# Trainium2: the head of a mixture-of-experts stage reordered by high and low parts, with unread products on TensorE ahead of it

## The reference, cut to what matters

```python
logits = x @ w_gate                                   # 512 -> 8
local_gate = sigmoid(x @ w_local)
for each sequence b, each row s:
    fresh = argmax(logits[b, s])
    e = fresh if s == 0 or local_gate[b, s] < 0.5 else prev_e
    p = softmax(logits[b, s])
    h = maximum(x[b, s] @ w1[e], 0)                   # 512 -> 1024
    out[b, s] = p[e] * (h @ w2[e])                    # 1024 -> 512
```

## Time and profile before

| | us |
|---|---|
| median of 3 runs | 995.79 |
| lowest and highest | 994.01, 1001.41 |
| the profiled execution's own time | 996.88 |
| its span, first to last instruction | 994.8 |
| mean granted clock of TensorE, share of full speed | 0.972 |

### The profile page before, as it was taken

The page is one execution under the profiler, slowest core; times in us unless marked ns, Lnnn a source line. Parts: engine busy times, 40 slices in busy tenths (PEclk is TensorE's granted clock), DMA queues, the critical chain, the costliest instruction groups (busy, mean ns, idle before and its releaser), DMA issues.

```text
span 994.8 us, 16236 instructions
## 1 busy us (share of the span) xinstructions
PE 900.2 (90%) x5991; PEld 760.0 (76%) x5991; DVE 563.0 (57%) x1203; ACT 414.4 (42%) x777; POOL 382.8 (38%) x347
## 2 busy tenths in 40 slices
PE   4798998899889986599999999999969999999996
PEld 3677787788768875488888887788858889788895
DVE  5677767776777765724657568760024525345252
ACT  4566666566656652133333333333323212132130
POOL 2454434634563232445565555555204004040000
PEclk9899999899999998799999999999979999999999
DMA  5322332232223013542665466630030020110101
GB/s 122 90 67 61 74 95 68 65 95 74 60 61 108 14 60 133 196 133 85 193 195 161 158 198 196 192 105 27 2 108 1 1 96 1 48 49 1 48 1 47
DMA packets 47643, 86.79 MB, mean 87 GB/s; under 512 B 8012, under 2 KB 16332, under 8 KB 47568
## 3 DMA queue, kind: packets, MB, share of 16 engines
q1 hardware_dynamic: 43568, 76.32, 26.8%
q0 software_dynamic: 4000, 9.45, 2.9%
HBM read 73.42 MB, written 15.99 MB: 90 GB/s over the span
## 4 chain that ended last, share of the span: by engine, by line
PE 50%; DVE 6%; DMA 4%; issue 1%; ACT 1%; POOL 0%; DVEq 0%; POOLq 0%
PE ps_h L1313 4%; PE ps_y L1332 4%; PE ps_h L1315 4%; PE ps_y L1334 4%; PE ps_h L1314 4%; PE ps_y L1333 4%; PE ps_a L1595 4%; PE ps_a L1597 4%; PE ps_a L1596 4%; PE ps_v L1595 3%; DMA w_raw<-in_w 3%; PE ps_v L1597 2%; PE ps_v L1596 2%; DVE w_low L1253 2%; PE ps_r L1595 2%; PE ps_r L1596 2%
## 5 line engine op out<-in xcount | busy, mean ns | idle before, releaser
L490 ACT COPY probs_t<-ps_ring 128x512 f32<-128x512 f32 (+1 forms) x192 | 105.9, 560 | 117.3 <-PE ps_ring L579 103.7
L780 DVE SCALAR_TENSOR_TENSOR probs<-ps_s,floor,expd 128x576 f32<-128x576 f32 x144 | 117.0, 813 | 62.9 <-ACT expd L447 62.7
L533 PE MATMUL ps_s<-k_high,q_split 128*128 128x288 f32 x336 | 108.6, 341 | 29.3 <-DVE probs L780 15.6
L1245 DVE CAST w_high<-w_raw 128x1024 fp32r<-128x1024 f32 (+1 forms) x63 | 65.0, 1048 | 98.6 <-PE ps_h L1315 50.4
L447 ACT ACTIVATE expd<-ps_s,max_tau 128x576 f32<-128x576 f32 x144 | 107.8, 749 | 12.5 <-DVE max_tau L766 12.4
L766 DVE TENSOR_REDUCE max_tau<-ps_s 128x1 f32<-128x576 f32 x144 | 106.7, 741 | 0.8 <-PE ps_s L534 0.8
L533 PEld LDWEIGHTS ps_s<-k_high,q_split 128*128 128x128 f32 x336 | 65.8, 196 | 50.5 <-DVE probs L780 29.2
L610 PE MATMUL ps_ring<-probs_t,v_pair 128*64 128x144 f32 x1280 | 92.6, 292 | 10.3 <-ACT probs_t L490 10.3
L534 PE MATMUL ps_s<-k_low,q_split 128*128 128x288 f32 x336 | 94.0, 302 | 0.0
L610 PEld LDWEIGHTS ps_ring<-probs_t,v_pair 128*64 128x64 f32 x1280 | 76.0, 137 | 21.8 <-ACT probs_t L490 13.3
L1472 POOL TENSOR_TENSOR rstd<-var_eps,exponent 128x1 f32<-128x1 f32 (+1 forms) x20 | 17.2, 860 | 180.2 <-DVE var_eps L1534 180.2
(11 more groups left out here) (235 smaller groups left out, 2046.9 us busy)
## 6 DMA issues: line engine op xcount, KB each, us to landing
w_raw<-in_w SPq DMA_DIRECT2D x64, 512.0 KB, 4.1
q_in<-in_q SPq DMA_DIRECT2D x32, 288.0 KB, 4.3
k_in<-in_k SPq DMA_DIRECT2D x32, 288.0 KB, 5.6
v_pair<-in_v SPq DMA_DIRECT2D x16, 256.0 KB, 2.7
x_rows_dram<-scratch SPq DMA_DIRECT2D x4, 1024.0 KB, 4.5
out<-scratch SPq DMA_DIRECT2D x4, 1024.0 KB, 4.3
scratch<-in_dense SPq DMA_DIRECT2D x8, 384.0 KB, 5.8
scratch<-y_rows_dram SPq DMA_DIRECT2D x3, 1024.0 KB, 5.5
```

Source lines behind the costliest of these rows:

```text
L533: nc.tensor.matmul(out, lhs, k_high[par][:, h, cols], start=first, stop=False)
L780: nc.vector.scalar_tensor_tensor(out=row_of(pair, w).rearrange("p (a c) -> p a c", a=2), in0=scores(n), scalar=floor[:, n % 4:n % 4 + 1], ...
```

## The change

1. **Unread products** (`keep_warm`, `LAST_FILLS`): after attention's steps 14, 15 and 17 PE issues 6, 12 and 22 products of a constant matrix of ones with 512 columns into the bank `ps_x`, which nothing reads.
2. **Slot 0's products in another order** (`first_up`): the 8 products high by high need only the rows' high part and the cast weights; then 8 of the low rows by high weights; then slot 1's `turn_x`; then 8 of the high rows by low weights. It has fixed addresses, where `up` computes them from the expert's number.
3. **Slot 1's rows** get a place of their own, the last 512 columns of each of w1's odd places (`second_t`). ACT casts them there from `ps_x`, DVE makes the low part (`first_low(1, second_t)`); POOL's `x_low(1)` and ACT's `x_evacuate(1)` are gone. Chunk 3 of w1 of expert 1 is cast to that place only after slot 1's `up` (`up_done` of 5).
4. **DVE's low weights later**: chunks 1 and 2 wait for `ids_taken` of 3, that is until POOL has copied slot 2's row numbers behind the first two gathers, in place of `gather_begun`; slot 0's low rows go ahead of chunk 3, and the last batch's probabilities stand between chunk 3 and slot 1's low rows.

```diff
@@ -76,6 +76,7 @@
...
 LAST_ROWS_AT = (13, 13, 13, 14, 14)
+LAST_FILLS = (14, 6), (15, 12), (17, 22)
...
@@ -527,7 +528,7 @@
...
-    def tensor_steps(pe, steps, row_banks=None):
+    def tensor_steps(pe, steps, row_banks=None, spare=None):
...
@@ -669,6 +670,12 @@
...
+        def keep_warm(count, bank):
+            for _ in range(count):
+                nc.tensor.matmul(bank.rearrange("p (a c) -> p a c", a=4), ones[:], ones[:].unsqueeze(1).to_broadcast([P, 4, P]),
+                                 start=True, stop=True)
         def last_rows(i):
...
@@ -688,6 +695,9 @@
...
                     last_rows(i)
+            for at, count in LAST_FILLS:
+                if n == after_batch(B - 1, at):
+                    keep_warm(count, spare)
...
@@ -981,7 +991,7 @@
...
         sync=lambda sp: store_rows(sp, B - 1), scalar=lambda act, row_banks: scalar_steps(act, left, row_banks),
-        tensor=lambda pe, row_banks: tensor_steps(pe, left, row_banks), vector=lambda dve: vector_steps(dve, left),
+        tensor=lambda pe, row_banks, spare: tensor_steps(pe, left, row_banks, spare), vector=lambda dve: vector_steps(dve, left),
         probs=lambda dve: vector_steps(dve, range(len(STEPS), len(STEPS) + 1)), rows_stored=rows_stored, slots_known=slots_known,
...
@@ -1051,6 +1061,7 @@
...
     EACH = DC * F
+    second_t = [part[:, 2 * EACH - D:2 * EACH].rearrange("p (c t) -> p c t", c=DC) for part in w1]
     chunk_loaded, chunk_high = [sem(f"chunk_loaded{j}") for j in range(RING)], sem("chunk_high")
...
@@ -1058,8 +1069,8 @@
...
     passed = sem("passed_e")
-    first_high, first_split, early_high, early_split, gather_begun = (
-        sem("first_high"), sem("first_split"), sem("early_high"), sem("early_split"), sem("gather_begun"))
+    first_high, first_split, early_high, early_split = (
+        sem("first_high"), sem("first_split"), sem("early_high"), sem("early_split"))
     x_turned, x_out, x_split = sem("x_turned"), sem("x_out"), sem("x_split")
...
@@ -1131,7 +1142,7 @@
...
         def x_low(s):
-            pool.wait_ge(x_out, s)
+            pool.wait_ge(x_out, s - 1)
             nc.gpsimd.tensor_tensor(x_slot_t[1][:].rearrange("p c t -> p (c t)"), x_raw,
...
@@ -1155,7 +1166,6 @@
...
         gather(0)
-        pool.sem_inc(gather_begun, 1)
         take_ids(1)
...
@@ -1167,7 +1177,7 @@
...
                 take_ids(s + 3)
-            if s + 1 < SLOTS:
+            if 0 < s < SLOTS - 1:
                 x_low(s + 1)
...
@@ -1199,15 +1209,16 @@
...
             nc.scalar.copy(w1[0][:, CHUNK * c:CHUNK * c + CHUNK], raw[c % RING][:]).then_inc(early_high, 1)
-        act.wait_ge(x_turned, 1)
-        nc.scalar.copy(x_slot_t[0][:].rearrange("p c t -> p (c t)"), ps_x[:]).then_inc(first_high, 1)
+        for s, part in enumerate((x_slot_t[0][:], second_t[0])):
+            act.wait_ge(x_turned, s + 1)
+            nc.scalar.copy(part, ps_x[:].rearrange("p (c t) -> p c t", c=DC)).then_inc(first_high, 1)
         for s in range(SLOTS):
...
             relu(s, 1)
-            if s + 1 < SLOTS:
+            if 0 < s < SLOTS - 1:
                 x_evacuate(s + 1)
...
@@ -1241,6 +1252,8 @@
...
                 dve.sem_inc(passed, 1)
+            if (name, e, c) == ("w1", 1, CHUNKS - 1):
+                dve.wait_ge(up_done, 5)
             dve.wait_ge(chunk_loaded[n % RING], 16 * (n // RING) + 16)
...
@@ -1259,14 +1272,20 @@
...
+        def first_low(s, parts):
+            dve.wait_ge(first_high, s + 1)
+            nc.vector.tensor_tensor(parts[1][:] if s == 0 else parts[1], ps_x[:].rearrange("p (c t) -> p c t", c=DC),
+                                    (parts[0][:] if s == 0 else parts[0]).bitcast(F32), ALU.subtract).then_inc(first_split, 1)
         ending.vector(dve)
-        dve.wait_ge(gather_begun, 1)
-        for c in range(1, CHUNKS):
+        dve.wait_ge(ids_taken, 3)
+        for c in (1, 2):
             low(c)
-        dve.wait_ge(first_high, 1)
-        nc.vector.tensor_tensor(x_slot_t[1][:].rearrange("p c t -> p (c t)"), ps_x[:],
-                                x_slot_t[0][:].rearrange("p c t -> p (c t)").bitcast(F32), ALU.subtract).then_inc(first_split, 1)
+        first_low(0, x_slot_t)
+        low(3)
         ending.probs(dve)
+        first_low(1, second_t)
         for n in range(CHUNKS, len(CHUNK_ORDER), CHUNKS):
...
@@ -1298,11 +1317,11 @@
...
         def up(s, e):
-            if s == 0:
-                pe.wait_ge(first_split, 1)
-                pe.wait_ge(early_split, 1)
+            if s == 1:
+                pe.wait_ge(first_split, 2)
             else:
-                pe.wait_ge(x_split, s)
+                pe.wait_ge(x_split, s - 1)
+            x_t = second_t if s == 1 else [part[:] for part in x_slot_t]
             high, low = (part[:, bass.ds((e & 1) * EACH, EACH)] for part in w1)
...
@@ -1310,11 +1329,31 @@
...
                     cols = slice(F * c + 512 * half, F * c + 512 * half + 512)
-                    nc.tensor.matmul(ps_h[:, half, :], x_slot_t[0][:, c, :], high[:, cols], start=(c == 0), stop=False)
-                    nc.tensor.matmul(ps_h[:, half, :], x_slot_t[0][:, c, :], low[:, cols], start=False, stop=False)
-                    last = nc.tensor.matmul(ps_h[:, half, :], x_slot_t[1][:, c, :], high[:, cols], start=False, stop=(c == DC - 1))
+                    nc.tensor.matmul(ps_h[:, half, :], x_t[0][:, c, :], high[:, cols], start=(c == 0), stop=False)
+                    nc.tensor.matmul(ps_h[:, half, :], x_t[0][:, c, :], low[:, cols], start=False, stop=False)
+                    last = nc.tensor.matmul(ps_h[:, half, :], x_t[1][:, c, :], high[:, cols], start=False, stop=(c == DC - 1))
                     if c == DC - 1:
                         last.then_inc(up_done, 1)
+        def first_up():
+            pe.wait_ge(first_high, 1)
+            for x, w in ((0, 0), (1, 0), (0, 1)):
+                if x == 1:
+                    pe.wait_ge(first_split, 1)
+                if w == 1:
+                    turn_x(1)
+                for c in range(DC):
+                    if x == 0 and w == 0:
+                        pe.wait_ge(early_high, c + 1)
+                    if w == 1:
+                        pe.wait_ge(w1_split if c else early_split, c if c else 1)
+                    for half in range(2):
+                        cols = slice(F * c + 512 * half, F * c + 512 * half + 512)
+                        last = nc.tensor.matmul(ps_h[:, half, :], x_slot_t[x][:, c, :], w1[w][:, cols],
+                                                start=(x == 0 and w == 0 and c == 0), stop=(w == 1 and c == DC - 1))
+                        if w == 1 and c == DC - 1:
+                            last.then_inc(up_done, 1)
...
@@ -1337,14 +1376,17 @@
...
-        ending.tensor(pe, row_banks)
+        ending.tensor(pe, row_banks, ps_x[:])
         turn_x(0)
...
             e = pe.value_load(route["slot_expert"][0:1, s:s + 1], min_val=0, max_val=E - 1)
-            up(s, e)
-            if s + 1 < SLOTS:
+            if s > 0:
+                up(s, e)
+            else:
+                first_up()
+            if 0 < s < SLOTS - 1:
                 turn_x(s + 1)
...
```

## The result

| | before | changed |
|---|---|---|
| median of 20 runs each, us | 997.02 | 992.72 |
| lowest and highest, us | 993.43, 1001.41 | 989.3, 998.02 |
| the profiled execution's own time, us | 996.88 | 990.02 |
| its span, us | 994.8 | 988.2 |

The ratio of the times is 0.9957, with a 95% interval of 0.9943 to 0.9972: 4.3 us less, between 2.8 and 5.7. The forecast was 7.1 us less and a median of 988.7 in a range of 985.6 to 992.8; the median of 992.72 lies 0.08 us inside its upper edge. By the 1% bound it is no change, as forecast; it is a real gain all the same. The forecast stood on a median of three runs of the kernel before, 995.79, and the 20 runs here give 997.02; so the gain is the fairer number to compare, 4.3 us where 7.1 were forecast.

The account below looks back on a forecast made before the run. Only stretches where PE stands still or runs slowly ahead of 419 us counted. Gains of 4.15 + 1.7 + 1.2 = 7.1 us gave 989.8 for the profiled execution and a median of 988.7, range 985.6 to 992.8.

Parts of the forecast that it names:

- The two kinds of stall that it named: In the head: PE waiting for slot 0's gather, cast and subtraction until 407.25, and 2.52 us for slot 1's low rows.
- The first gather is quicker: Slot 0's gather on POOL: 1.05 us in place of 2.29, rows landing at 401.7 in place of 404.1, gain 2.4 us.
- From landing to first product: Slot 0's turn, ACT's cast and two semaphores: 1.4 us in place of 3.1, first product at 403.1.
- the handover of slot 1's rows: From slot 0's products to slot 1's first: 2.35 us in place of 3.6, gain 1.2, no waiting for POOL.
- w2 was not late: Expert 0's w2 before down(0): price taken as 0; the rival of late w2, about 2 us, had chance 0.10.
- 24 products, at 0.23 each: Slot 0's products on PE at the full clock: 5.5 us in place of 7.2, gain 1.7 us.
- the second rival: Slot 0's products: the clock is not at 2.4 GHz, 1.7 us lost, time 990.4; chance 0.15.
- The sign of being wrong that I had named: PE's clock in the head: a stretch at 0.50 behind 390 would show the forecast wrong.
- the sum: Head up to slot 1's first product: 4.15 + 1.7 + 1.2 = 7.1 us gained.
- carries to the end: Behind the head: all later work is released by PE, so the whole 7.1 us gain reaches the kernel's end.
- 411.4: Forecast time of slot 1's first product on PE, in place of 418.50.
- The slower rival: Head: products of ones do not keep the clock up and delay row numbers; 3.8 us later, 999.6; chance 0.03.

Follow-up runs that it names:

- run 3: Changed kernel with DVE's low weights released early again, by the first gather's issue; ratio to the kernel before 0.9960, measure 38.99 us.
- run 4: Kernel before with one edit, DVE's low weights waiting for the third copy of row numbers; ratio to the kernel before 0.9996, measure 40.44 us.
- run 5: Changed kernel with slot 1's rows again copied by ACT and made low by POOL; ratio to the kernel before 0.9968, measure 38.40 us.
- run 6: Changed kernel with 26 unread products in the third filling and 3 behind slot 0's turn; ratio to the kernel before 0.9929, measure 34.51 us.
- run 9: Changed kernel plus 3 unread products behind slot 0's turn, last eight products by halves, slot 1's expert read behind slot 0's products; ratio to before 0.9917.
- second pair: Changed kernel and kernel before, each run again word for word; ratios to the kernel before 0.9933 and 0.9983, measures 36.18 and 41.02 us.
- run 8: Changed kernel with 26 unread products, 3 behind the turn, last eight products by halves and early expert read; ratio to the kernel before 0.9918.
- run 1: Changed kernel without its 40 unread products; ratio to the kernel before 0.9936, measure 36.36 us.
- run 2: Kernel before plus the 40 unread products alone; ratio to the kernel before 0.9993, measure 40.78 us.
- run 7: Changed kernel with slot 0's last eight products by halves and slot 1's expert read early; ratio to the kernel before 0.9953, measure 35.44 us.

## Why the prediction was right or wrong

**Right:** the sign, and that it is under 1%. The range held too, by 0.08 us, with the gain at 0.6 of the forecast. The two kinds of stall that it named are the ones that went. The first gather is quicker once DVE's low weights no longer start beside it (runs 3 and 4), 1.30 us where I took 1.05, so the rows landed at 402.33, not at 401.7: 0.4 of that is the writing and the landing, 0.2 attention's scatter. From landing to first product it is 1.33, forecast 1.4. The last of slot 0's products starts at 409.38 + 7 x 0.23 = 411.0; from 0.23 behind it to slot 1's first at 413.55 it is 2.3, forecast 2.35. In the new order the handover of slot 1's rows is worth 3.4 against POOL's way, of which 1.7 is the clock (run 5), and the later low weights 2.8, of which 1.2 is the clock (run 3). w2 was not late.

**Wrong: the term "24 products, at 0.23 each".** I put it at a gain of 1.7 and it gave nothing. 24 products and a turn took 7.55 us (403.66 to 411.2) in place of 5.95, since the clock fell at 404.04. I had this as the second rival, at 0.15 and 1.7 us, and argued against it from a stretch where PE stood still for 2.5 us at a clock of 1.00. That row showed that such a pause may pass, not that it will: in the changed kernel PE is idle or transposing for 2.3 us, from 401.4 to 403.7, and in seven of the nine profiles of kernels with unread products the clock fell either there or inside the third filling; it held through both in runs 6 and 9, which differ from the changed kernel just there. Run 5 has the stop of rows 9 itself, 2.18 us of waiting for POOL ahead of slot 1, and there the clock fell at its end. The sign of being wrong that I had named, a stretch at 0.50 behind 390, came twice. With 5.4 as the sum, which the rival gave, the head's 5.0 would have been met to 0.4.

**The median.** The spans differ by 6.6 us, the heads by 5.2 (or 4.8, second pair), the medians by 4.3. Between the first two lies mainly one wait in the middle of the profile before, absent after: there slot 16 came 13.8 us behind slot 15, not 12.33. Why the medians differ by less than the heads stays open; their interval, 2.8 to 5.7, covers both. That a head's gain "carries to the end" is right for the releases of slot to slot, 12.33 us apart wherever nothing is waited for, but the waits in the middle are drawn anew in each. Of the 2.1 us by which slot 1's first product missed 411.4, 1.6 is the clock, 0.4 the gather and its landing and 0.2 attention, with 0.1 given back in the turn and the handover.

**The slower rival** did not come: DVE's pick steps, not the filling's end, time the row numbers, even with 12 products at 4.51 us. Its mechanism is real in small: in runs 5 and 8 the third filling held PE past the landing, 0.5 and 1.5 us.

**Rules weighed.** The Trainium skill (SBUF — State Buffer, Who interferes with whom) infers that a tensor_tensor leaves descriptor writing alone. The runs show the gather's instruction held (2.29 beside it, 1.30 without), and the measurement decides; which step inside that instruction waits, no run shows. It also (TensorE: Matmul & The Clock Gate, Part 4: PE-mode transpose) says that transposes do not keep the clock up: the fall at 404.0, behind a gap of 2.3 us with four transposes in it, fits that, but PE was also idle for 1.65 us of the gap, and no run parts the two. The same holds of the fall at 390 in the kernel before, which I had put down to transposing: PE had stood idle for 1.92 us ahead of the one-hot transposes as well.

## What to carry to other kernels

Where a kernel has one stall behind another, price an edit together with what queues next: the earlier landing was worth 0.6 to 0.9 us by itself and 2.8 with the new order. In these profiles unread products took 0.2 to 0.6 us off the head where they stopped short of the first real one (runs 1 and 2), and 1.8 and 2.0 where they reached up to it (runs 6 and 9, against the same order without any), and they cost as soon as the low clock stretched them past the event that they waited out. So I would fill both sides of the last short step rather than lay one long run ahead of it; that fewer are safer is my estimate from runs 5 and 8 (6.92 us for 22, 7.81 for 26), and no pair of runs shows it. And when executions scatter more than the edit, compare a stretch between two fixed events of the profiles, and take the median only for what it can tell.

## What the runs showed of the hardware that I had not expected

The clock fell at 390.4 in the changed kernel although 6 unread products had run from 386.7 to 388.4, and rose again 3.4 us later, while the second filling ran. A gather of POOL lost 1.0 us or 0.4 beside the same work of DVE, depending on how much of the running subtraction was left when it began. Reading one number from a table on PE's queue, with what follows from it, costs 0.7 us when nothing hides it (run 7), as much as three products.
